# Layer 2 of a two-layer block pipeline runs five chunks behind layer 1 instead of six

## What is computed

```python
def _moe_ref(x, w_in, w_out, a, b):
    h = x @ w_in
    h2 = h * h
    h3 = h2 * h
    P = a[0] + a[1] * h + a[2] * h2 + a[3] * h3
    Q = 1.0 + np.abs(b[0]) * np.abs(h) + np.abs(b[1]) * h2
    g = P / (Q + 1e-06)
    return (g @ w_out).astype(np.float32)
...
def _moe2_ref(x, w_in, w_out):
    h = x @ w_in
    relu6 = np.clip(h + 3.0, 0.0, 6.0)
    g = h * relu6 / 6.0
    return (g @ w_out).astype(np.float32)
```

## Time and profile before

| | |
|---|---|
| time, median of 3 runs | 1278.91 us (1278.4 to 1279.31) |
| the profiled execution: time, span | 1279.6 us, 1277.8 us |
| PE, DVE, ACT, POOL busy, share of the span | 94%, 93%, 93%, 87% |
| mean granted TensorE clock | 0.982 |

### The profile page before, as it was taken

How to read it: one execution, slowest core, us unless ns; L and a number is a source line. 1 busy time by engine, 2 the same in 40 slices (tenths; PEclk the granted TensorE clock), 3 DMA queues, 4 the chain that set the end, 5 groups by cost and what they waited for, 6 DMA issues and landing times.

```text
span 1277.8 us, 19186 instructions
## 1 busy us (share of the span) xinstructions
PE 1195.1 (94%) x5128; PEld 966.7 (76%) x5128; DVE 1193.3 (93%) x1910; ACT 1186.2 (93%) x2221; POOL 1105.4 (87%) x859
## 2 busy tenths in 40 slices
PE   2456899999999999999999999999999999999998
PEld 1334688888878888888878888788888888888876
DVE  6688999999999999999999999999999999999932
ACT  3878899999999999999999999999999999999954
POOL 5878889899998989899898989999898989965554
PEclk9779899999999999999999999999999999999999
DMA  5453223231322232131332214123222312000000
GB/s 167 104 120 79 70 55 65 64 66 32 78 60 54 50 82 61 36 75 45 69 72 57 51 53 83 33 57 73 62 50 66 63 34 46 13 17 13 2 13 13
DMA packets 61461, 73.57 MB, mean 58 GB/s; under 512 B 15912, under 2 KB 42280, under 8 KB 61096
## 3 DMA queue, kind: packets, MB, share of 16 engines
q1 hardware_dynamic: 61352, 72.35, 24.4%
HBM read 56.44 MB, written 8.01 MB: 50 GB/s over the span
## 4 chain that ended last, share of the span: by engine, by line
PE 64%; DVE 19%; issue 10%; ACT 6%; DMA 1%; SPq 0%; POOLq 0%; POOL 0%; ACTq 0%; DVEq 0%
PE h L683 7%; PE h L687 6%; PE h L684 6%; PE h L685 6%; PE h L686 6%; PE acc L691 6%; PE acc L695 6%; PE acc L692 6%; PE acc L693 6%; PE acc L694 6%; DVE early L1076 4%; DVE early L1070 3%; DVE early L1101 3%; DVE early L1064 3%; DVE q_recip L1085 2%
## 5 line engine op out<-in xcount | busy, mean ns | idle before, releaser
L620 POOL TENSOR_TENSOR g_lo<-early,g_hi 128x512 fp32r<-128x512 f32 x256 | 333.2, 1302 | 94.1 <-ACT g_hi L877 85.9
L629 POOL TENSOR_TENSOR g_lo<-late,g_hi 128x512 fp32r<-128x512 f32 x256 | 333.3, 1302 | 23.7 <-ACT g_hi L897 23.7
L683 PE MATMUL h<-x_hi,w_in_hi 128*128 128x512 f32 x512 | 208.3, 407 | 50.6 <-DVE early L1101 48.1
L1109 DVE SCALAR_TENSOR_TENSOR late<-late,h 128x512 f32<-128x512 f32 x256 | 174.4, 681 | 37.9 <-ACT late L888 35.6
L691 PE MATMUL acc<-g_hi,w_out 128*128 128x512 f32 x512 | 202.2, 395 | 5.4 <-DVE late L1121 3.0
L684 PE MATMUL h<-x_lo,w_in_hi 128*128 128x512 f32 x512 | 202.1, 395 | 0.0
L685 PE MATMUL h<-x_hi,w_in_lo 128*128 128x512 f32 x512 | 202.0, 394 | 0.0
L686 PE MATMUL h<-x_tail_hi,w_in_tail 128*128 128x512 f32 x512 | 201.8, 394 | 0.0
L687 PE MATMUL h<-x_tail_lo,w_in_tail 128*128 128x512 f32 x512 | 201.5, 394 | 0.0
L692 PE MATMUL acc<-g_hi,w_out 128*128 128x512 f32 x512 | 200.8, 392 | 0.0
L693 PE MATMUL acc<-g_lo,w_out 128*128 128x512 f32 x512 | 200.4, 391 | 0.0
(11 more groups left out here) (87 smaller groups left out, 2394.8 us busy)
## 6 DMA issues: line engine op xcount, KB each, us to landing
mix_w<-mix_weights SPq DMA_DIRECT2D x75, 192.0 KB
mix_w<-mix_weights SPq DMA_DIRECT2D x75, 144.0 KB
x_win<-in_x SPq DMA_DIRECT2D x15, 393.0 KB, 3.4
mix_w<-mix_weights SPq DMA_DIRECT2D x60, 96.0 KB
mix_w<-mix_weights SPq DMA_DIRECT2D x60, 72.0 KB
out_y<-late SPq DMA_DIRECT2D x16, 256.0 KB, 2.0
x_tail_hi<-tail_hi SPq DMA_DIRECT2D x60, 64.0 KB, 2.0
x_tail_lo<-tail_lo SPq DMA_DIRECT2D x60, 64.0 KB, 2.0
```

Source lines behind the costliest of these rows:

```text
L620: nc.gpsimd.tensor_tensor(g1_lo[p][:, :], neg_g[p], g1_hi[p][:, :].bitcast(F32), ALU.subtract).then_inc(g1_lo_ready, 1)
L629: nc.gpsimd.tensor_tensor(g2_lo[p][:, :], gate[p], g2_hi[p][:, :].bitcast(F32), ALU.subtract).then_inc(g2_lo_ready, 1)
L683: pe.matmul(out[:, :], w_hi[:, cols], hi[:, :], start=True, stop=False)
```

## The change

Five numbers become smaller by one.

```diff
-SHIFT = 6
+SHIFT = 5
...
-        X2_TAIL_HI = 5
-        SUMS2 = 8
+        X2_TAIL_HI = 4
+        SUMS2 = 7
...
-        X2_TAIL_LO = 6
+        X2_TAIL_LO = 5
```

## The result

20 runs of each kernel give 1280.6 us (1280.39 to 1281.33) for the changed one against 1278.57 us (1277.79 to 1279.47) for the one before: a ratio of 1.0016, 95% interval 1.0009 to 1.0023, or +2.0 us. The forecast was +2.4 us, with "same", within 0.2%, the likeliest of the three. The change makes four numbers smaller by one, those of its diff; the text ahead of it counts five.

A forecast was written before the change was run, and what follows sets the result against it. TensorE was taken as the bound, VectorE close behind. 9 x 0.37 + 5 x 0.36 = 5.1 us lost in the middle, 2.7 gained at the ends: +2.4 on 1278.9, 1281.3 us, range 1277.6 to 1284.0.

The forecast's parts named there:

- TensorE is the bound: Segments 1 to 14: TensorE sets the pace at 4.53 us a plain step; rival that VectorE is the bound, chance 0.08.
- VectorE 0.16 us a step faster: Plain steps: VectorE takes 4.37 us against TensorE's 4.53, so it gains 0.16 us in each.
- its reserve gone at step 5: VectorE's lead in ending L1101 before TensorE needs its bank is wiped out by the stall behind step 3's sum.
- The ends, -2.7 us: Start and end of the kernel: one 2.83 us step goes, a 4.02 us step becomes 4.53; gain 2.3 to 2.83.
- L915, 0.21 to 0.29 us a segment: ScalarE's rounding in step 4: delays L1085 by 0.29 us; 0.21 remain in segments like 4, 0.29 like 5.
- L1127 a step earlier: VectorE's result addition: still lengthens its step by 0.96 us, with one plain step less before it, 0.16 us less reserve.
- The reading as a wait for ScalarE: At L1127: part of the 0.96 us is a wait for ScalarE's copy; some 0.1 us a block would vanish, 1.4 in all.
- the model that the Trainium skill gives: At L1127: an instruction starting in another 32-partition group is held until earlier Vector work has finished; cost stays 0.96 us.
- The sum for a segment: Middle of the kernel: 0.37 us lost in each of nine segments like 4, 0.36 in five like 5, 5.1 us.
- the refill: TensorE's step behind a stall: takes 4.71 us instead of 4.53, about 0.18 us on top of the wait.
- GpSimd at nothing: L646 ends by 430.7, layer 2 in of step 6 starts at 432.15: 1.4 us spare, no cost; rival's chance 0.05.
- the stall at steps 4 and 5: Behind the block's sum at step 3: through ScalarE's three copies and VectorE back to TensorE; left as it is.

The follow-up runs named there:

- experiments 4 to 6: Short reductions (L990) of odd segments moved to other steps, on the kernel before, the changed one and one with seven chunks: 1276.24 to 1292.10 us.
- experiment 7: Changed kernel with the tail's rounding and low part left at steps 5 and 6, layer 2 still a chunk sooner: 1328.68 us, 1.0397.
- experiments 4 and 5: L990 in steps 2, 9, 10, 12: 1291.96 us (kernel before), 1292.10 (changed); in 1, 2, 9, 10: 1278.50 (before), 1281.04 (changed), 1279.04 (seven chunks).
- experiment 6: L990 of segments 3, 5, 7, 9 in steps 1, 2, 9, 10, segment 1 unmoved: 1276.24 us on the kernel before, 1278.45 on the changed one.
- experiment 4, first kernel: Kernel before with the odd segments' four reductions (L990) in steps 2, 9, 10, 12 instead of 4, 6, 8, 10: 1291.96 us, 1.0105.

## Why the prediction was right, point by point

*TensorE is the bound, VectorE 0.16 us a step faster, its reserve gone at step 5.* Right: experiments 4 to 6 change only the places of VectorE's work and move the steps. In segments 4 and 5 of all 13 profiles the L1101 that step 4 needs ends 0.95 to 1.52 us ahead of it, and the one that step 5 needs 0.05 to 0.08 us. In these two segments the change moved steps 4 and 5 by 0.04 us at most.

*The ends, -2.7 us.* Right in size. The last stretch gave 2.95, 0.12 more than the one step of 2.83; where these 0.12 come from I did not follow. The start, to segment 1, can't be read to better than a microsecond: five chunks began it at 181.5 to 182.4 us in four other profiles (183.04 in experiment 7, whose wait falls into it too), six at 181.4 to 181.9 in four. The net of the ends is 2.0 - 4.8 = -2.8 from the runs. The same reckoning of five against six chunks, whole time less middle, gives -2.9 in experiments 4 and 5 and -2.3 in experiment 6, and seven against six +2.3. So the range of 2.3 to 2.83 holds to 0.1 us, but the choice of 2.7 in it is not confirmed.

*L915, 0.21 to 0.29 us a segment.* Right in size: alone 0.18 and 0.31 in segments 4 and 5, +3.4 us in all. The link was read wrong. I took the 0.15 us from L869's end to L1085 for the distance at which VectorE waits. VectorE waits for L888, one operation earlier, at a distance of 0.03: in step 5 of the kernel before, too, L888 ended at 435.05 and L1109 began at 435.08. The room on this link was 0.26 - 0.03 = 0.23, and L888 came 0.48 us later, which makes 0.25. On the link that I used it was 0.22 of room and 0.51, 0.29 late. The two are nearly the same because L1085 keeps its distance from L1109; that the wrong link gave a good number was luck.

*L1127 a step earlier.* Its 0.96 us moved along unchanged (5.34 us a step). The place cost 1.4 us by difference; 5.1 less 3.3 for L915 had left 1.8. The reading as a wait for ScalarE, which would have dropped, can't be judged in segment 4, where ScalarE's L922 ends 0.09 to 0.10 us ahead of L1127 in both kernels. Segment 5 of the changed kernel refutes it, first ScalarE, then VectorE:

```profile
515.45 0.59 ACT L922 ACTIVATE late<-acc 64x512 f32<-64x512 f32 x1
```

```profile
515.69 0.69 DVE L1070 TENSOR_TENSOR early<-early,h 128x512 f32<-128x512 f32 x1
516.41 0.69 DVE L1127 SCALAR_TENSOR_TENSOR late<-acc,late 64x512 f32<-64x512 f32 x1
```

L922 has ended 0.37 us before L1127, and the seam is 0.03 all the same. Where L922 really is late (experiment 4, first kernel, segments 2, 4, 6 and 8), L1127 begins 0.03 after its end and the seam is 0.20. The seams of L1127 agree with the model that the Trainium skill gives ("VectorE: DVE Perf Modes", "Two Vector instructions with no wait between them"); no run here tries another partition.

*The sum for a segment.* +0.37 and +0.36 forecast, +0.32 and +0.38 measured in segments 4 and 5; step 8 of segment 4 at 5.03 against 5.05. (From the terms that the prediction lists for segment 5, 0.62 - 0.18 - 0.1, comes 0.34, not 0.36.) The middle is 4.8 instead of 5.1 us. Over all 14 the nine segments without reductions grew by 0.26 to 0.39, 0.34 on average, 0.03 short of the forecast: the refill is 0.14 after the change (4.67) where I took over the 0.18 of one row. The five with them grew by 0.35 on average.

*GpSimd at nothing.* Right, with 1.5 us to spare. Experiment 7 shows the price when the cover is gone: in half of the segments larger than I had put it, because of the clock.

*Untested:* whether step 5 would keep wiping out the reserve if ScalarE's copies at step 3 were shorter. All kernels here have the stall at steps 4 and 5.

## What to carry to other kernels

Where two engines are close to full, look for the place at which the faster one loses its reserve, and count what it has to do from there to its next large piece; a per-block operation that costs VectorE under 0.1 us in one step (L915 in step 5: a step of 4.45 instead of 4.37 us) can cost 0.25 us one step earlier. A shorter pipeline lag pays once, at the ends (2.3 to 2.9 us here); what it squeezes is paid in each of 14 blocks. Before moving work, look at who consumes it and what stands behind that consumer in its queue: the same reductions cost 13 us in one set of steps and gained 2 in another.

## What was not expected of the hardware

A matmul group can be delayed with no matmul starting late: the weight load waits for the same semaphore, and one that came 0.25 us late cost 0.16 us in the step after it. An operation on 64 partitions cost VectorE 0.96 us where a full one takes 0.60 to 0.66 from start to start, with three seams of 0.03 us; the one ahead of it stayed when ScalarE had been done for 0.37 us. After a wait of about 3.1 us TensorE ran at 0.51 of its clock for 3.4 us in segment 4 of experiment 7 and at 1.00 in segment 5; after waits of 0.3 to 0.6 us in the changed kernel the windows of the segments show 1.00.
